# Attention scores in 64x64 quarters, one score buffer, and a down product cut in twelve shares

## Time and profile before

| | us |
|---|---|
| median of 3 runs (lowest, highest) | 548.64 (548.2, 553.62) |
| span of the profiled execution | 544.8 |
| PE matmuls busy | 512.0 (94%) |
| DVE busy | 277.0 (51%) |
| ACT busy | 248.3 (46%) |
| POOL busy | 160.9 (30%) |

### The profile page before, as it was taken

The page is one execution under the profiler, slowest core; times in us unless marked ns, Lnnn a source line. Parts: engine busy times, 40 slices in busy tenths (PEclk is TensorE's granted clock), DMA queues, the critical chain, the costliest instruction groups (busy, mean ns, idle before and its releaser), DMA issues.

```text
span 544.8 us, 10551 instructions
## 1 busy us (share of the span) xinstructions
PE 512.0 (94%) x4036; PEld 485.4 (89%) x4036; DVE 277.0 (51%) x490; ACT 248.3 (46%) x638; POOL 160.9 (30%) x154
## 2 busy tenths in 40 slices
PE   5869699999989999899999998999999999999997
PEld 4759689999979999899998987998999899989997
DVE  4888975528957249765288517444123411342020
ACT  4837573418765058744187327326212621252121
POOL 3573642302443005423034015045004410441030
PEclk9999989999999999999999999999999999999999
DMA  7991002540023600125500100000200020002002
GB/s 208 284 286 55 10 16 58 148 123 0 19 49 87 173 19 0 29 60 170 185 31 0 40 2 0 1 1 1 88 0 0 0 87 0 0 0 87 1 0 88
DMA packets 33132, 32.76 MB, mean 60 GB/s; under 512 B 20818, under 2 KB 22354, under 8 KB 32724
## 3 DMA queue, kind: packets, MB, share of 16 engines
q1 hardware_dynamic: 30852, 28.23, 17.4%
q10 hardware_dynamic: 2256, 4.21, 2.3%
HBM read 27.71 MB, written 4.72 MB: 60 GB/s over the span
## 4 chain that ended last, share of the span: by engine, by line
PE 41%; issue 32%; POOL 13%; DVE 10%; ACT 2%; DMA 0%; POOLq 0%; DVEq 0%; SPq 0%; ACTq 0%
PE dense L358 28%; PE dense L548 11%; POOL ar L1006 6%; POOL vp L994 6%; DVE tmp L824 4%; DVE qk L911 2%; PE score L371 1%; POOL vrstd L1041 1%; DVE tmp L835 1%; DVE wr L830 1%; PE pt_ps L381 1%; ACT qk L711 1%; DVE negmax L776 0%; DMA qk<-q_blocks 0%; ACT vp L749 0%
## 5 line engine op out<-in xcount | busy, mean ns | idle before, releaser
L358 PE MATMUL dense<-ar,wr 128*128 128x288 f32 x1152 | 162.5, 299 | 9.7 <-POOL ar L1006 6.6
L358 PEld LDWEIGHTS dense<-ar,wr 128*128 128x128 f32 x1152 | 155.8, 190 | 12.1 <-ACT tmp L628 5.5
L358 PE MATMUL dense<-xr,wr 128*128 128x288 f32 x1152 | 155.4, 296 | 2.6 <-ACT tmp L731 2.1
L358 PEld LDWEIGHTS dense<-xr,wr 128*128 128x128 f32 x1152 | 153.2, 188 | 3.6 <-ACT tmp L731 2.4
L824 DVE SCALAR_TENSOR_TENSOR tmp<-tmp,taps 128x576 f32<-128x576 f32 x64 | 68.6, 1072 | 22.1 <-ACT tmp L634 21.0
L1006 POOL TENSOR_TENSOR ar<-tmp,ar 128x576 fp32r<-128x576 f32 x32 | 43.1, 1352 | 124.0 <-ACT ar L645 124.0
L548 PE MATMUL dense<-wr,ar 128*128 128x288 f32 x448 | 60.1, 295 | 0.0
L603 ACT ACTIVATE vp<-score,bias 128x128 f32<-128x128 f32 x144 | 50.8, 367 | 19.8 <-DVE bias L779 19.7
L1054 POOL TENSOR_TENSOR ar<-vp,ar 128x576 fp32r<-128x576 f32 x16 | 25.1, 1567 | 117.7 <-ACT ar L741 117.7
L548 PEld LDWEIGHTS dense<-wr,ar 128*128 128x128 f32 x448 | 59.7, 188 | 0.0
L994 POOL TENSOR_TENSOR vp<-vp,recip 128x512 f32<-128x512 f32 x36 | 37.4, 1040 | 64.8 <-DVE recip L800 64.8
(11 more groups left out here) (70 smaller groups left out, 477.8 us busy)
## 6 DMA issues: line engine op xcount, KB each, us to landing
vp<-v_rows SPq DMA_DIRECT2D x36, 256.0 KB, 2.9
qk<-q_blocks SPq DMA_DIRECT2D x72, 64.0 KB, 2.5
out_t<-vp SPq DMA_DIRECT2D x16, 288.0 KB, 2.1
qk<-k_t SPq DMA_DIRECT2D x3, 1152.0 KB, 6.8
x2keep<-w_in ACTq DMA_DIRECT2D x2, 1024.0 KB, 6.6
qk<-w_in SPq DMA_DIRECT2D x1, 2048.0 KB, 7.6
x2keep<-w_out ACTq DMA_DIRECT2D x1, 1280.0 KB, 7.2
vp<-w_spatial_t SPq DMA_DIRECT2D x1, 1152.0 KB
```

The source lines that it names most:

```text
L358: last = mm(dst, stationary(a, t), moving(c, t), start=(t == 0 and n == 0), stop=(t == (of or len(tiles)) - 1 and n == 2))
```

## The change

It has four parts. The scores are computed on quarters of the array, 64 rows by 64 columns: four mask matmuls (head half h by pair group c, 256 columns each) and eight products (one per head), with q loaded as it is, without the zeros. Heads h lie in one bank each, so the single buffer `score` has two banks; the first batch alone uses `dense[1]` for its odd steps. From the second batch on, scores of a step wait until all exponentials of the step before are done. The down product becomes 64 pieces of three matmuls, laid in twelve shares behind the steps 0 to 11. The loops over batches are written out. The order of the probabilities in `prob` changes with it (heads first), so `values` reads other slices. q is loaded like k, in three parts for the first batch and whole for the others. POOL builds a 64-wide identity in both halves and the mask first, and the 128-wide identity for the transposes behind them. `score_view` is `dense[1]` for odd steps of the first batch and `score` otherwise.

```diff
-            def scores(j, g, start):
-                s = score[j % 2]
+            def scores(j, g, b):
+                s = score_view(j, b)
...
-                if later(ring_free(j, g, start)):
-                    pe.wait_ge(exp_done, ring_free(j, g, start))
-                m = mask[:, 1 if j == 0 else 0, :].unsqueeze(1).to_broadcast([P, PAIRS, P])
-                mm(s[:, :, :], ident_b[:, :], m, start=True, stop=False, skip_group_check=True)
-                for i in range(PAIRS):
-                    last = mm(s[:, i, :], q_diag[:, j % 3, i, :], k_sb[:, i, window], start=False, stop=True,
-                              skip_group_check=True)
+                free = g - 1 if b == 0 else g
+                if later(free):
+                    pe.wait_ge(exp_done, free)
+                for c in range(2):
+                    for h in range(2):
+                        rows = slice(h * HD, (h + 1) * HD)
+                        m = mask[rows, 1 if j == 0 else 0, :].unsqueeze(1).to_broadcast([HD, 2, P])
+                        mm(s[c * HD:(c + 1) * HD, h, :], ident_b[rows, :], m, start=True, stop=False,
+                           skip_group_check=True)
+                for i in range(2):
+                    for c in range(2):
+                        for h in range(2):
+                            rows = slice(h * HD, (h + 1) * HD)
+                            last = mm(s[c * HD:(c + 1) * HD, h, i * P:(i + 1) * P],
+                                      q_sb[rows, 2 * c + i, j * WINDOW:(j + 1) * WINDOW],
+                                      k_sb[rows, 2 * c + i, window], start=False, stop=True, skip_group_check=True)
                 last.then_inc(score_done, 1)
...
+        def down_pieces(early):
+            pieces = [(d, c, t) for d in range(2) for c in range(2) for t in range(early)]
+            pieces += [(0, c, t) for ts in (range(early, FT - 1), range(FT - 1, FT)) for c in range(2) for t in ts]
+            pieces += [(1, c, t) for c in range(2) for t in range(early, FT)]
+            return pieces + [(d, c, t) for d in range(2, KT) for c in range(2) for t in range(FT)]
...
+        SHARES = [5, 10, 5, 5, 4, 4, 5, 5, 5, 6, 5, 5]
...
-            with pe.Fori(0, B - 1) as b:
-                for kind, n in ORDER:
-                    if kind == "down":
-                        down_unit(n, b, x2_kept, KT * b + 1, FT - 3)
-                    else:
-                        attention_step(n, b + 1)
+            pe.wait_ge(exp_done, NB)
+            up(0, started=True)
+            for b in range(0, B - 1):
+                for t in range(STEPS):
+                    attention_step(t, b + 1)
+                    if t < len(SHARES):
+                        for n in range(ENDS[t] - SHARES[t], ENDS[t]):
+                            down_piece(n, b, PIECES, EARLY, x2_kept, KT * b + 1)
...
-                sp.dma_start(k_sb, k[b + 1]).then_inc(k_loaded, 16)
-                for kind, j in FETCH:
-                    (load_q if kind == "q" else load_v)(j, NB * b + NB + j, b + 1)
+                sp.dma_start(k_sb, k[b + 1]).then_inc(qk_loaded, 16)
+                sp.dma_start(q_sb, q[b + 1]).then_inc(qk_loaded, 16)
+                for j in range(NB):
+                    load_v(j, NB * b + NB + j, b + 1)
```

More of the change, by code:

```diff
@@ L33, in later @@
 def later(value):
-    return not isinstance(value, int) or value > 0
+    return value > 0
 def program(nc, q, k, v, w_in, conv_w, w_out, w_in2, w_sp, b_sp, w_out2, out):
@@ L241, in program, with score_view @@
         OUT_FIRST = 3
[L244 to L252, removed]
+        def score_view(j, b):
+            t = dense[1] if b == 0 and j % 2 else score
+            return t[:, :, 0:2 * P]
+        def down_pieces(early):
[3 more added lines that the diff above has]
+            return pieces + [(d, c, t) for d in range(2, KT) for c in range(2) for t in range(FT)]
+        EARLY = FT - 3
+        PIECES = down_pieces(EARLY)
+        SHARES = [5, 10, 5, 5, 4, 4, 5, 5, 5, 6, 5, 5]
+        ENDS = [sum(SHARES[:i + 1]) for i in range(len(SHARES))]
+        assert ENDS[-1] == len(PIECES) and len(SHARES) == STEPS - 1
+        LAST_PIECE = {d: max(i for i, p in enumerate(PIECES) if p[0] == d) for d in range(KT)}
+        WHOLE = {t: [d for d in range(KT) if (ENDS[t - 1] if t else 0) <= LAST_PIECE[d] < ENDS[t]]
+                 for t in range(len(SHARES))}
         def raw_out(t):
@@ L283, in _ @@
         def _(sp):
[L284 to L291, removed]
             def load_v(j, g, b):
@@ L339, in _ @@
             sp.dma_start(raw_out2[0], w_out2_t[:, 0:GT // 2, :]).then_inc(out2_loaded, 16)
-            with sp.Fori(0, B) as s:
+            for s in range(0, B):
                 for d in range(KT):
@@ L583, in _ @@
             pe.wait_ge(late_lo, N_SPATIAL)
-            with pe.Fori(0, B - 1) as s:
+            for s in range(0, B - 1):
                 spatial_tiles(s)
@@ L596, in _, with exponentials @@
         def _(act):
-            def exponentials(j, g, start):
+            def exponentials(j, g, b):
                 if later(g - 2):
@@ L602, in exponentials @@
                 for i in range(PAIRS):
-                    last = nc.scalar.activation(prob[:, j % 3, i, :], score[j % 2][:, i, :], ACT.Exp,
+                    last = nc.scalar.activation(prob[:, j % 3, i, :],
+                                                score_view(j, b)[:, i // 2, i % 2 * P:(i % 2 + 1) * P], ACT.Exp,
                                                 bias=bias[:, j, i:i + 1], scale=SCALE,
@@ L616, in attention_step @@
                 if t < NB:
-                    exponentials(t, NB * b + t, NB * b)
+                    exponentials(t, NB * b + t, b)
             def up(b):
@@ L672, in _ @@
             act.wait_ge(split_lo_out, N_PIECES)
-            with act.Fori(0, B - 1) as b:
+            for b in range(0, B - 1):
                 for t in range(STEPS):
@@ L756, in _ @@
                 late_high(i)
-            with act.Fori(0, B - 1) as s:
+            for s in range(0, B - 1):
                 uv_high(s)
@@ L862, in _ @@
             up(0, range(OUT_FIRST, N_PIECES))
[L863 to L868, removed]
+            for b in range(0, B - 1):
+                for t in range(STEPS):
+                    attention_step(t, b + 1)
+                    for d in WHOLE.get(t, ()):
                         keep_x2(d, b)
@@ L954, in _ @@
             dve.wait_ge(late_lo, len(late))
-            with dve.Fori(0, B - 1) as s:
+            for s in range(0, B - 1):
                 for d in range(GT):
@@ L986, in _ @@
                     pool.wait_ge(built, done)
+            pl.memset(minus_half[:, :], -0.5).then_inc(consts, 1)
+            pl.memset(ident[:, :], 0.0).then_inc(built, 1)
+            pool.wait_ge(built, done + 1)
+            pl.affine_select(out=ident[:, :], in_=ident[:, :], compare_op=ALU.not_equal, fill=1.0, base=0,
+                             pattern=[[-1, P]], channel_multiplier=1).then_inc(consts, 1)
             pl.memset(vrstd[:, :], 1.0).then_inc(consts, 1)
@@ L1018, in _ @@
             up(0, range(OUT_FIRST, N_PIECES))
-            with pool.Fori(0, B - 1) as b:
+            for b in range(0, B - 1):
                 for j in range(NB):
@@ L1057, in _ @@
             v_steps(0)
-            with pool.Fori(0, B - 1) as s:
+            for s in range(0, B - 1):
                 uv_low(s)
```

130 lines of the change are left out of this document (54 added, 76 removed).

## The result

The changed kernel takes 560.13 us (median of 4 runs, 557.75 to 561.61), the kernel before in the same comparison 548.43 (4 runs, 548.2 to 553.62): a ratio of 1.0203 [1.017, 1.0235], 11.7 us more.

What follows compares the result with a forecast made beforehand. The prediction took TensorE, busy nearly all the time, as the bound. Three turns at +5.7 us, less 1.5 for the first batch, made +15.7 on 548.6: 564 us, range 551 to 573.

Steps and rivals of the forecast that it cites:

- s: PE's time for one step's scores on quarters: 1.09 us against 1.20 before, bounds 0.64 and 2.3.
- The idle stretch at the turn: PE idles before scores 1 at each of three turns until exponentials 0 end: about 7 us, 5 in the first.
- The clock: Granted clock falls to half behind the idle stretch, slowing scores 1 and the next down matmuls: 2.0 us per turn.
- my first rival: Sixteen score records fill all four quarters at once: s = 0.64, total 553.5 us (+4.9), within 1%; chance 0.27.
- the sum of the prediction: Whole kernel: three turns at 8s - 3.0 each, less 1.5 for the first batch, +15.7 us with s = 1.09.
- The first batch: Small q loads become three issued at once, shortening the wait before scores 4: -1.5 us, bounds 0 and -4.
- 8 x 0.67 - 5.0: Loss per turn before the clock, forecast as 8s - 5.0 us from PE's work left after the idle stretch.
- One buffer behind the turn: Later steps with a single score buffer: PE stays the longer one by 0.2 us, so it costs nothing there.
- s + 2.78: PE's own work in a step of four down pieces, in us; 0.4 more with five.
- s + 2.6: Shortest step with one buffer, in us: scores, then bias and exponentials until PE is released.
- Written-out loops at nothing: Batch loops written out on all engines: taken as 0 us, with 4.6 in all as the upper bound.
- Around the span: Time of a run outside the profiled span: 3.8 us, taken as unchanged.

Runs made afterwards that it cites:

- The wait alone: The kernel before, with scores 1 waiting for exponentials 0 from batch 1 on and nothing else changed: 571.27 us, ratio 1.039.
- the covered turn: Changed kernel with scores 1 of every batch in `dense[1]`, down tile 0 laid first, tile 1 behind exponentials 1, new share sizes: 538.3 us, ratio 0.9802 to the kernel before.
- Filling the stretch alone: Changed kernel with 38 matmuls of unused result in PE's idle time before scores 1 of each turn: 554.95 us, ratio 1.0102 to the kernel before.
- the order experiment: Changed kernel with both score products of a quarter next to each other instead of the four quarters in turn: 558.61 us, ratio 1.0176 to the kernel before.

## Why the prediction was right, and where it was wrong

The forecast of 564 us (551 to 573, slower with 0.79) stands 3.9 above the measured 560.13. The place and the size of the main loss were right. That the sum came within 4 us is partly luck: s was 10.1 us too dear, and other terms, most of them priced at nothing, made up for more than half of it.

**The idle stretch at the turn: right.** About 7 us were forecast, 5 in the first turn; 7.20, 7.22 and 5.51 came, ended by ACT's exponentials. The wait alone gave +22.6 us, and the covered turn took back 21.8.

**The clock: right, small error.** It fell in all three turns, and cost 1.21 - 0.67 = 0.54 at the scores and 5.80 - 30 x 0.139 = 1.63 at the 30 matmuls, 2.2 per turn against 2.0. Filling the stretch alone took back 5.2 of the 6.5 us, with the third turn's fall still there. One reading in my text was off: slices at 0.80 and 0.78 put the lower level from 66.6 to 73.4 and not from 66.4 to 73.6, so the clock fell 2.9 us after PE stopped. Nothing of the sum changes by it.

**What s is: this step failed.** I took s = 1.09, from records that start in program order, so that four quarters bring no more than two halves. The trace shows 0.67 to 0.68, and the pace of four records per 0.11 us. The other order of the products should have cost another 24 us by program order; it cost 0.07 a step in the rows and nothing that the runs' times show. This is my first rival's mechanism, all four quarters at once, and its s = 0.64. The mis-sized term is 8 x 3 x (1.09 - 0.67) = 10.1 us too much. The Trainium skill ("TensorE: Matmul & The Clock Gate", part 3) says that matmuls start and end in strict program order; the pace and the order experiment don't agree with the price that I drew from it. The trace doesn't tell one record of a product from the other, so whether first records pass second ones or both run together stays open.

**Then why not the rival's 553.5?** With s = 0.67 the sum of the prediction is 3 x (5.4 - 3.0) - 1.5 = +5.6. What is missing to +11.7 lies mostly in terms that I had priced at nothing:

- The table load. Written out, the loop lets it stand behind the wait for the bias: exponentials 0 end 0.44 us later after the start of the turn (157.49 - 146.90 = 10.59, before 152.53 - 142.38 = 10.15). Times 3: 1.3 us. In the kernel before, the same edit cost 3.3; how much of it came through the load isn't clear of noise.
- The shares. 147 matmuls of the down product lie in ten shares behind step 1, where the kernel before had six. In the second turn they take 21.7 us by their rows, against my 147 x 0.139 = 20.4, which is also what they took before: 1.3 more. Of this 0.4 is the one buffer (see below). In the rest a share of 15 takes 2.14 to 2.19, where one before a mask took 2.09 (154.54 to 156.63); each is now left for matmuls of another tile shape. Against it, the nine transposes take 3.7 us instead of 3.9, as all of them have down matmuls behind them. The twelve shares were not tried alone, so that price is read from the rows, not shown by an experiment.
- The first batch. Scores 4 start at 13.82 as forecast (15.72 before), and the up stage at 36.78 instead of 37.68. But behind a wait of 1.70 us at 35.87 the clock was at 0.50 from 37 to 39, and the turn began at 62.80, not earlier than 62.38. In the kernel with the covered turn the clock held from 36 to 38 (1.00), and the turn began at 61.13, 1.25 earlier. So 1.25 of the 1.5 was there, and the clock took it in this execution.

For the second turn these give 8 x 0.67 - 5.0 = 0.4, the clock's 2.2, 0.4 for the table and 1.3 - 0.2 for the shares with the buffer's wait and the transposes: 4.1, as the trace has it. Three turns give 11.8 (measured). The profiled executions differ by 2.2 more, of which 0.4 lie ahead of the first turn and 1.4 in the third layer. There 48 matmuls follow a wait of 2.15 us, and take 361.61 - 353.69 = 7.92 us at a clock of 0.50 from 354 to 356, against 347.73 - 341.25 = 6.48 in the profiled execution of before. The change touches that place only by the written-out loops, and they are not the reason: the kernel with the wait alone, which keeps its hardware loops, has the same fall there in its profiled execution, behind a wait of 2.15 us at 363.99 (0.50 from 365 to 367).

PE in the changed kernel at that place:

```profile
353.69 8.08 PE L354 MATMUL dense<-xr,wr 128*128 128x288 f32 x48 [2.15 <-ACT tmp L723]
361.61 0.56 PE L539 MATMUL dense<-wr,ar 128*128 128x288 f32 x3
```

**One buffer behind the turn: right, but not quite at nothing.** PE's matmuls show no wait for exponentials behind scores 1. The weight loads do (PEld), short ones, since a matmul's record is its latency and hides them:

```profile
PEld score L369 <- ACT vp L594: 8.5, 5, 7.4
...
174.61 0.21 ACT L594 ACTIVATION_READ_ACCUMULATOR vp<-score,bias 128x1 f32 x1
...
174.88 0.11 PEld L369 LDWEIGHTS score<-mask,ident_b 64*64 64x64 bf16 x4 [0.35 <-ACT vp L594]
```

Scores 3, 4 and 5 of the second turn (167.87, 171.24, 174.88) all start 0.06 us after the last exponentials' record of the step before. It costs 0.12, 0.12 and 0.17, read against shares of equal size that nothing holds: the four pieces from 171.24 to 174.88 took 3.64 us, s + 2.97, and the next four 3.47, s + 2.80, where I had s + 2.78. I had allowed up to 0.2 on three steps. In the third of them the exponentials started only at 173.32, behind the values' copy (L603) and 0.30 us more for the transposes (L388), which my s + 2.6 left out. From scores 6 on nothing is held.

**Written-out loops at nothing: wrong,** by 3.3 us as an edit by itself (1.5 to 5.3 by the interval of its ratio). Instruction fetches rose from 16 packets to 35 and 0.4% of the DMA engines; nothing ties the time to them.

**Around the span** lie 1.8 us and not 3.8: the profiled execution of before was simply faster than the median.

**Where the gain of the change is.** The wait costs 22.6 us, the written-out loops 3.3, and the whole change 11.7. So the quarters, the early loads and the shares together bring 14 (by difference, if the parts add). The cheaper scores alone are 8 x 3 x (1.20 - 0.67) = 12.7 of it on paper.

## What to carry to other kernels

Price a removed buffer at the place where a batch turns, by what stands in the queue behind the instruction that now waits; where that stretch outlasts the work left ahead of the wait, look for any bank that is idle just then, since one borrowed use at the turn was worth 22 us here. Price the clock with it: behind an idle stretch what follows can run at half speed. And try one reordering of a disputed series of matmuls before its cost is argued.

## What the runs showed of the hardware

- Two-record fp32 products on 64 x 64 quarters ran four records at a time, 0.108 us per four records of 128 columns (0.43 us for sixteen more). With the two products of a quarter next to each other a step's scores took 0.74 us instead of 0.67.
- The granted clock fell behind waits of PE of only 1.7 to 2.2 us (1.70 at 35.87 and 2.15 at 353.69 in the changed kernel, 2.21 at 153.66 with written-out loops), and held behind equal ones (2.22 at 230.21 with written-out loops, 1.72 at 37.07 and 2.14 at 341.25 before). What decides isn't settled by these runs.
- The function table of ACT was loaded behind the semaphore wait of the activation that needs it where the loop was written out (0.54 us after the wait began), and ahead of it in the hardware loop. An activation of one column without a wait of its own put it forward, to 0.70 us after the copy before it.
- Going from the quarters to the next tile shape (values or transposes) cost about 0.11 us, read from 0.54 for sixteen records up to the next product against 0.43 for sixteen more.
